# Two PSUM banks for the value sums, q and k turned in halves through one bank, the outcome's product on GpSimd, and no loop over heads

## What is computed

```python
q_bits = (einsum(q, proj) > 0)               # 6 bits for each token; k_bits alike
mask = q_bucket[..., :, None] == k_bucket[..., None, :]
scores = where(mask, q @ k.T / 8, -1e9)
attn = exp(scores - max); attn = attn / (sum(attn) + 1e-09)
x = attn @ v
h = maximum(maximum(x @ w1, x @ w2), x @ w3) @ w_out       # 512 -> 768 -> 512
return elu(h @ w_in) @ w_out2                              # 512 -> 2048 -> 512
```

## Time and profile before

| | before |
|---|---|
| median of 3 runs | 746.4 us (745.79 to 746.6) |
| the profiled execution | 744.61 us |
| its span, first to last instruction | 742.8 us |
| granted TensorE clock, mean | 0.989 |
| busy: PE, PEld, DVE, ACT, POOL | 97%, 83%, 51%, 57%, 50% |
| attention, until PE's first feed-forward matmul | 280.33 us |

### The profile page before, as it was taken

The page is one execution under the profiler, slowest core; times in us unless marked ns, Lnnn a source line. Parts: engine busy times, 40 slices in busy tenths (PEclk is TensorE's granted clock), DMA queues, the critical chain, the costliest instruction groups (busy, mean ns, idle before and its releaser), DMA issues.

```text
span 742.8 us, 10492 instructions
## 1 busy us (share of the span) xinstructions
PE 720.6 (97%) x3469; PEld 618.8 (83%) x3469; DVE 380.8 (51%) x615; ACT 424.5 (57%) x821; POOL 367.8 (50%) x333
## 2 busy tenths in 40 slices
PE   6899999999999979999999999999999999999998
PEld 5699999999998868888888888788888888888886
DVE  6768888988888844322222221243344433444333
ACT  4488989989898982221222121355555555555553
POOL 5377888888888871021110010254545444454442
PEclk8799999999999999999999999999999999999999
DMA  7656456464545000211000010133334333343331
GB/s 150 156 112 137 97 129 146 92 135 97 123 107 136 0 1 21 65 43 44 21 22 1 21 34 31 54 104 98 89 111 143 102 97 94 105 142 108 92 100 56
DMA packets 79317, 63.44 MB, mean 85 GB/s; under 512 B 29080, under 2 KB 68712, under 8 KB 79272
## 3 DMA queue, kind: packets, MB, share of 16 engines
q1 hardware_dynamic: 77416, 62.47, 33.0%
q10 hardware_dynamic: 1856, 0.40, 0.3%
HBM read 40.91 MB, written 3.15 MB: 59 GB/s over the span
## 4 chain that ended last, share of the span: by engine, by line
PE 60%; DVE 0%; ACT 0%; issue 0%
PE banks L781 14%; PE banks L783 14%; PE banks L782 14%; PE banks L1128 6%; PE banks L1124 6%; PE banks L1125 6%; DVE g_sb L1067 0%; DVE g_sb L1063 0%; DVE out_sb L1037 0%; ACT gh L1022 0%; ACT neg L1017 0%
## 5 line engine op out<-in xcount | busy, mean ns | idle before, releaser
L934 POOL TENSOR_TENSOR wl<-raw,wh 128x512 fp32r<-128x512 f32 (+2 forms) x104 | 143.5, 1398 | 301.7 <-ACT wh L950 301.7
L351 POOL TENSOR_TENSOR p_lo<-probs,p_hi 128x384 fp32r<-128x384 f32 x192 | 197.0, 1043 | 53.9 <-ACT p_hi L419 53.0
L781 PE MATMUL banks<-xh,wh 128*128 128x512 f32 x408 | 158.9, 389 | 0.5 <-PEq L126 0.5
L782 PE MATMUL banks<-xl,wh 128*128 128x512 f32 x408 | 158.8, 389 | 0.0
L783 PE MATMUL banks<-xh,wl 128*128 128x512 f32 x408 | 158.7, 389 | 0.0
L556 DVE TENSOR_REDUCE half_max<-banks 128x1 f32<-128x384 f32 x192 | 99.5, 547 | 27.7 <-PE banks L677 26.8
L418 ACT ACTIVATE probs<-banks 128x384 f32<-128x384 f32 x192 | 95.1, 495 | 26.2 <-PE banks L692 22.5
L419 ACT ACTIVATE p_hi<-banks 128x384 fp32r<-128x384 f32 x192 | 95.1, 496 | 0.0
L1063 DVE TENSOR_SCALAR g_sb<-banks 128x512 f32<-128x512 f32 x48 | 33.2, 692 | 120.1 <-ACT neg L1017 120.1
L781 PEld LDWEIGHTS banks<-xh,wh 128*128 128x128 f32 x408 | 76.6, 188 | 17.0 <-issue 0.9
L783 PEld LDWEIGHTS banks<-xh,wl 128*128 128x128 f32 x408 | 76.5, 188 | 16.0
(11 more groups left out here) (119 smaller groups left out, 1189.4 us busy)
## 6 DMA issues: line engine op xcount, KB each, us to landing
operands<-wh SPq DMA_DIRECT2D x36, 384.0 KB, 7.0
raw<-in_moe_w_in SPq DMA_DIRECT2D x48, 256.0 KB, 2.7
raw<-in_moe_w_out SPq DMA_DIRECT2D x48, 256.0 KB, 2.8
raw<-in_moe_w SPq DMA_DIRECT2D x18, 256.0 KB, 3.9
wl<-wh SPq DMA_DIRECT2D x9, 384.0 KB, 6.7
v_raw<-in_v SPq DMA_DIRECT2D x16, 192.0 KB, 2.5
out_dram<-out_sb SPq DMA_DIRECT2D x12, 256.0 KB, 2.1
q_raw<-in_q SPq DMA_DIRECT2D x15, 192.0 KB, 3.4
```

The source lines that it names most:

```text
L351: pool.tensor_tensor(p_lo[:, at, :], probs[:, step % RING, :], p_hi[:, at, :].bitcast(FP32), ALU.subtract).then_inc(pl_done, 1)
L781: pe.matmul(out, sh, mh, start=first, stop=False)
L782: pe.matmul(out, sh, ml, start=False, stop=False)
L934: pool.tensor_tensor(wl[:, j, at:at + cols], raw[:, j, at:at + cols], wh[:, j, at:at + cols].bitcast(FP32), ALU.subtract).then_inc(w_ready, 1)
```

## The change

1. `pv_ps` becomes two banks: the first half of every head goes into one, the second into the other. The first L706 of a half waits for the copies of the half before the last (the `o_read` counts go down by 2).
2. That bank comes from `misc`: from slot 1 on, q and k are turned, rounded, subtracted and projected through one bank (`single`), in halves of three transposes. PE turns q's halves at steps 0 and 3, k's at 5 and 8. ACT rounds each half (128x384) after the exponentials of the following step (1, 4, 6, 9). DVE subtracts the four halves before maxima 4, 7 and 11, and at the slot's end. Each transposing half waits until DVE has read the half before it; the projection of k waits for the bits of q.
3. The outcome's product moves from DVE (`divide`) to POOL, behind the last `p_lo` of the slot.
4. The loop is gone: all 22 slots are written out, and all counts are constants.

```diff
-TP_AT, HASH_AT = (0, 6), (3, 6)
+TP_AT, HASH_AT = ((0, 3), (5, 8)), (3, 6)
+LOW_AT = ((4, 7), (11, None))
...
-def all_slots(eng, emit):
-
-    for s in range(FIRST_SLOT, LOOP_FROM):
+def all_slots(emit):
+
+    for s in range(FIRST_SLOT, LAST_SLOT + 1):
         emit(Slot(s))
-    with eng.Fori(0, LOOP_TIMES) as g:
-        for j in range(GROUP):
-            emit(Slot(LOOP_FROM + j, g))
...
-        pv_ps = banks[:, RING + 2, :]
+        pv_ps = [banks[:, RING + 2 + i, :] for i in range(2)]
         misc = banks[:, RING + 3:, :]
+        single = banks[:, RING + 4, :]
...
+                if s.has_unit:
+                    pool.wait_ge(inv_done, s.count(2, -2))
+                    unit = (s.off - 2) % 4
+                    pool.tensor_tensor(x[:, unit, :], x[:, unit, :], inv[:, unit, :], ALU.mult).then_inc(x_done, 1)
...
+            def high_half(s, x, n, half):
+
+                if half == 0:
+                    act.wait_ge(t_half, s.count(1, n - 1))
+                else:
+                    act.wait_ge(t_ready, s.count(1, 3 + n))
...
+                act.activation(hi[x][:, half, :], single[:, 0:HALF], ACT.Copy
+                               ).then_inc(hi_done if half else hi_half, 1)
...
+                    for i, name in enumerate("qk"):
+                        if s.has_tp and s.off > FIRST_SLOT + 2 and step - 1 in TP_AT[i]:
+                            high_half(s, name, i + 1, TP_AT[i].index(step - 1))
...
+            def low_half(s, x, n, half):
+
+                if half == 0:
+                    dve.wait_ge(hi_half, s.count(1, n - 1))
+                else:
+                    dve.wait_ge(hi_done, s.count(1, 3 + n))
+                dve.tensor_tensor(lo[x][:, half, :], single[:, 0:HALF], hi[x][:, half, :].bitcast(FP32), ALU.subtract
+                                  ).then_inc(lo_done if half else lo_half, 1)
...
-                if s.has_unit:
-                    divide(s)
...
+            def transposes_half(s, x, n, half):
+
+                src = q_raw if x == "q" else k_raw
+                par = (s.off + 3) // 2 % 2
+                if half == 1:
+                    pe.wait_ge(lo_half, s.count(1, n - 1))
+                elif n == 1:
+                    pe.wait_ge(q_in[par], s.count(8, 56 - 16 * par))
+                    pe.wait_ge(bits_done, s.count(1, 3))
+                else:
+                    pe.wait_ge(k_in[par], s.count(8, 56 - 16 * par))
+                    pe.wait_ge(lo_done, s.count(1, 4))
+                for t in range(TH):
+                    last = pe.transpose(single[:, t * P:(t + 1) * P],
+                                        src[:, par, half * TH + t, :, :].rearrange("p a d -> p (a d)"), ident[:])
+                last.then_inc(t_ready if half else t_half, 1)
...
+                if s.off > FIRST_SLOT + 3 and n == 2:
+                    pe.wait_ge(bits_done, s.count(1, 3))
...
-                    wait(pe, o_read, s.count(4, -2 if step < LAG else 0))
+                    wait(pe, o_read, s.count(4, -4 if step < LAG else -2))
...
-                out, kept = pv_ps[:, 0:HALF], (STEPS * s.off + step - LAG) % KEPT
+                half = at // T
+                out, kept = pv_ps[half][:, 0:HALF], (STEPS * s.off + step - LAG) % KEPT
```

More of the change, by code:

```diff
@@ L99 @@
     has_hash = property(lambda s: not s.odd and -2 <= s.off <= HEADS - 4)
-def all_slots(eng, emit):
-    for s in range(FIRST_SLOT, LOOP_FROM):
+def all_slots(emit):
+    for s in range(FIRST_SLOT, LAST_SLOT + 1):
         emit(Slot(s))
-    with eng.Fori(0, LOOP_TIMES) as g:
-        for j in range(GROUP):
-            emit(Slot(LOOP_FROM + j, g))
[L109 to L115, removed]
 def wait(eng, sem, count):
-    if not isinstance(count, int) or count > 0:
+    if count > 0:
         eng.wait_ge(sem, count)
@@ L266, in emit @@
                 if s.has_max:
-                    head = held(sp, s.count(1, 1))
+                    head = s.count(1, 1)
                     wait(sp, vl_done, s.count(1))
@@ L277, in emit @@
                 if s.has_hash:
-                    split = s.count(1, 4) if s.g is None else sp.to_reg(s.count(1, 4))
+                    split = s.count(1, 4)
                     wait(sp, st_ready, s.count(STEPS) if s.off >= 2 else 0)
@@ L297, in emit @@
                         sp.wait_ge(consts, 14)
-                    both = s.count(1, 4) if s.g is None else sp.to_reg(s.count(1, 4))
+                    both = s.count(1, 4)
                     sp.wait_ge(bits_done, both)
@@ L371, in outcome @@
                 act.wait_ge(pv_ready, s.count(2, half - 1))
-                act.activation(x[rows, unit, :], pv_ps[0:D, 0:HALF], ACT.Copy).then_inc(o_read, 1)
-                act.activation(inv[rows, unit, :], pv_ps[D:P, 0:HALF], ACT.Copy).then_inc(o_read, 1)
+                act.activation(x[rows, unit, :], pv_ps[half][0:D, 0:HALF], ACT.Copy).then_inc(o_read, 1)
+                act.activation(inv[rows, unit, :], pv_ps[half][D:P, 0:HALF], ACT.Copy).then_inc(o_read, 1)
+            def high_half(s, x, n, half):
[3 more added lines that the diff above has]
+                    act.wait_ge(t_ready, s.count(1, 3 + n))
+                for a in range(2):
+                    act.wait_ge(spread1[a], s.count(SPREAD1 / 2, 1.5 * SPREAD1))
+                    act.wait_ge(spread2[a], s.count(SPREAD2 / 2, 1.5 * SPREAD2))
+                act.activation(hi[x][:, half, :], single[:, 0:HALF], ACT.Copy
+                               ).then_inc(hi_done if half else hi_half, 1)
             def high(s, x, n):
@@ L503, in take_bits @@
                 elif x == "q":
-                    last = dve.tensor_scalar(bits[:, 0, :], misc[:, 0, 0:HALF], 0.0, half_bits[:], ALU.is_gt,
+                    bank = misc[:, 0, :] if s.off == FIRST_SLOT + 3 else single
+                    last = dve.tensor_scalar(bits[:, 0, :], bank[:, 0:HALF], 0.0, half_bits[:], ALU.is_gt,
                                              ALU.subtract)
                 else:
-                    last = dve.tensor_scalar(bits[:, 1, :], misc[:, 1, 0:HALF], k_above[:], k_times[:], ALU.is_gt,
+                    last = dve.tensor_scalar(bits[:, 1, :], single[:, 0:HALF], k_above[:], k_times[:], ALU.is_gt,
                                              ALU.mult)
@@ L545, in emit @@
                         reciprocals(s, 1)
-                    if n == MAX_BEFORE[TP_AT[0] + 3] and s.has_tp and s.off != FIRST_SLOT + 2:
+                    if s.off == FIRST_SLOT and n == 0:
                         low(s, "q", 1)
+                    for i, name in enumerate("qk"):
+                        if s.has_tp and s.off > FIRST_SLOT + 2 and n in LOW_AT[i]:
+                            low_half(s, name, i + 1, LOW_AT[i].index(n))
                     if n == MAX_BEFORE[HASH_AT[0] + 1] and s.has_hash:
@@ L704, in weigh @@
                 pe.wait_ge(pl_done, s.count(STEPS, step - LAG + 1))
-                out, kept = pv_ps[:, 0:HALF], (STEPS * s.off + step - LAG) % KEPT
+                half = at // T
+                out, kept = pv_ps[half][:, 0:HALF], (STEPS * s.off + step - LAG) % KEPT
                 pe.matmul(out, v_hi[:, h % 2, kt, :], p_hi[:, kept, :], start=(kt == 0), stop=False)
                 pe.matmul(out, v_hi[:, h % 2, kt, :], p_lo[:, kept, :], start=False, stop=False)
-                pe.matmul(pv_ps[0:D, 0:HALF], v_lo[:, h % 2, kt, :], p_hi[:, kept, :], start=False, stop=False
+                pe.matmul(pv_ps[half][0:D, 0:HALF], v_lo[:, h % 2, kt, :], p_hi[:, kept, :], start=False, stop=False
                           ).then_inc(pv_step, 1)
@@ L713, in weigh @@
                         pe.wait_ge(empty_done, s.count(1, 1))
-                    half = at // T * HALF
-                    pe.matmul(out, total[:, h % 2, :], empty[:, h % 2, half:half + HALF], start=False, stop=True
+                    pe.matmul(out, total[:, h % 2, :], empty[:, h % 2, half * HALF:(half + 1) * HALF], start=False, stop=True
                               ).then_inc(pv_ready, 1)
@@ L727, in emit @@
                     for i, x in enumerate("qk"):
-                        if s.has_tp and step == TP_AT[i] and s.off != FIRST_SLOT + 2:
+                        if s.off == FIRST_SLOT and step == 6 * i:
                             transposes(s, x, i + 1)
+                        if s.has_tp and s.off > FIRST_SLOT + 2 and step in TP_AT[i]:
+                            transposes_half(s, x, i + 1, TP_AT[i].index(step))
                         if s.off == FIRST_SLOT + 2 and x == "q" and step == 3:
```

40 lines of the change are left out of this document (19 added, 21 removed).

## The result

The changed kernel takes 756.19 us (four runs, 755.26 to 757.9) beside 746.1 us of the kernel before on the same chip: a ratio of 1.0127, 95% interval 1.0106 to 1.0148. It is slower by 10 us. The forecast was 746.8 us and the range ended at 751.0.

What follows compares the result with a forecast made beforehand. PE, busy 97% of the span, was taken as the bound, with ACT, DVE and POOL near their limits mid-attention. +4.9 - 1.3 - 3.2 = +0.4 us on the profiled 744.61 gave 745.0, on the median 746.8; range 740.5 to 751 us.

Steps and rivals of the forecast that it cites:

- What is removed: Slots 1 to 12: two banks end PE's holds for the copies, 0.86 us a pair of slots, 5.2 us for six.
- Groups of transposes: On PE, four groups instead of two: about 0.09 us for each change of kind, 0.18 us a pair, 1.1 for six.
- The three waits of the halves: Odd slots, steps 3, 5 and 8: PE waits for the half before to be read, 0.2 to 0.3, 0.7, 0.4 us.
- w: Added waits of the halves in an odd slot, restarts included: 1.5 us, between 0.9 and 2.1; six make 9.0 us.
- the chain of step 5: k's first half: from PE's scores 4 to DVE's subtraction 2.5 us, PE's matmuls 1.8; a wait of 0.7, the surest.
- Neither is next in line there: Middle of attention: splitting adds 0.3 us a pair on ACT, with 2.2 of 30 us free, and as little on DVE.
- The longer chain: Rival, chance 0.20: `v_lo` and maxima ahead of the low half before maximum 4 double the first wait; 750.4 us.
- has lost its product: Argument for the covered-waits rival (chance 0.30; 741.4 us at w = 0.6): DVE's freed 0.94 us brings it sooner in each chain.
- cost nothing: POOL's added product, 1.04 us a slot, fits into 4.2 of 30 us free; if POOL were late, 0 to 1 us a pair.
- The loop: Writing out the loop over slots is worth 0 to 0.2 us; taken as 0.
- Slots 12 to 14: Without copy waits a slot falls from 15.0 to 14.3 or 14.5 us, limited by ACT and POOL; gain about 1.3 us.
- The end of attention: Slot 15 without PE's 2.11 us hold: POOL bounds, six `p_lo` 6.25 us plus 0.4 for DVE's subtraction; gain 3.2 us.

## Why the prediction was wrong

- **What is removed: right.** L706 no longer waits for the copies; the 0.86 us a pair are gone.
- **Groups of transposes: right.** 0.09 us for each change of kind, as taken.
- **The three waits of the halves: right in place, order and size.** Forecast 0.2 to 0.3, 0.7 and 0.4 us; lost start to start 0.29, 0.85 and 0.49, restart included, together 1.63. w was taken as 1.5. The argument that the chain of step 5 starts from PE itself was the sound one; the rounding one step sooner took nearly all three waits away, which shows that ACT's place in the step made them.
- **"Neither is next in line there": the step that failed.** It was said of ACT and DVE by their busy time, 28 and 26 of 30 us. But order decides, not share: DVE had 108.7 us of work in 133, less than before (109.5 in 124), and PE waited for its maxima 16 times between 40 and 290 us. `v_lo` is not mentioned in the part-by-part working at all; it was neither added nor moved by the change, and so its slack against `v_hi` and against the ring of maxima was not read. Both were in the trace of before: in its slot 8, `v_hi` ends at 153.63 and `v_lo` begins at 153.79, a slack of 0.16 us. The three terms 1.63, 0.18 and -0.86 make +0.95 us a pair; the maxima add 0.45, 0.96 and 0.10, 2.46 in all, against +2.35 measured. The prediction had put the maxima's term at nothing.
- **The longer chain, the rival priced 750.4 us, had the right place and too small a price.** It named DVE before maximum 4 with `v_lo` and the maxima ahead. It looked only at the halves of the odd slots. The wait falls on the ring of maxima itself, which is there in every slot, and it is the even slot that pays the larger part (0.96 of 1.41 us). `v_lo` one place later gives 9.8 us, 1.8 of them in slots 12 to 14; without this wait the time is 746.4 beside a forecast of 746.8. That close a match is in part luck: slots 12 to 14 then gain 2.0 us where 1.3 were forecast, and the end gains 2.3 where 3.2 were.
- **DVE "has lost its product": the freed 0.94 us did not help.** It stood for sooner turns of DVE. In the runs the product left DVE's queue at the slot's end but lengthened `v_lo` by 0.3 us (0.93 to 1.23) in its middle.
- **The product on POOL, "cost nothing": wrong in this order, right in another.** 2.9 us over the product on DVE, through DVE and not through ACT's wait for `probs`. With `v_lo` one place later it gains 2.7 us. The price of the operation itself, 1.04 us, was right (1.014). But the 0.94 us for L597 on DVE, with which the prediction compared it, is a mean over two kinds: in the middle of attention half of them take 0.54 to 0.56 us and the others 1.23 to 1.33, waiting beside POOL. Alone the product is 0.54 us on DVE, so POOL takes nearly twice as long, and the prediction's "nearly the same" was wrong.
- **The loop: right,** nothing.
- **Slots 12 to 14: 14.80 us instead of 14.3 to 14.5.** The same wait for maxima takes 0.8 and 0.5 us there; without it they take 13.9, so the limit by POOL that was argued, 14.2 us a slot, was too high: POOL is then busy for 27.29 of 27.81 us, 13.6 a slot.
- **The end of attention: 22.75 us after slot 14,** 2.3 us gained of 3.2. POOL sets the end, as argued, and its six `p_lo` begin as far behind slot 14 as forecast (14.45 us, forecast 14.37). But they take 7.44 us, not 6.65. DVE's large subtraction begins 0.01 us ahead of them, and the first `p_lo` takes 2.61 us: it waits for all of it, 1.6 us where 0.4 was put, of which the other five give back some at 0.97 us each. That is 0.8 of the missing 0.9 us. Of the gain itself a part is the clock: before, PE's hold of 2.11 us was followed by a fall, and the stretch had a mean granted clock of 0.93; after, it has 1.00.

```profile
285.35 1.74 DVE L613 TENSOR_TENSOR wl<-raw,wh 128x1536 fp32r<-128x1536 f32 x1
285.36 7.44 POOL L341 TENSOR_TENSOR p_lo<-probs,p_hi 128x384 fp32r<-128x384 f32 x6 [0.76 <-ACT p_hi L425]
```

- **The start.** PE waits 1.6 us once for a DMA of `bits` on the way to slot 1. The same distance varies from 15.2 to 20.3 us among the kernels here, with no edit near it; what sets it stays open. In the profiled executions shown it is 3.5 us longer after (18.65) than before (15.17); the odd slot's 1.87 us and the DMA wait of 1.6 make that up. The wait may be part of why these two are 13.3 us apart and the medians 10.1; the profiled run after is also the longest of its four.

## What to carry to other kernels

An edit that removes a wait lets the engine that had it run ahead, and what stops it next need not be the busiest engine; here it was the instruction that stands in front of the one it now waits for: read, for each ring, what is queued ahead of its release and how late that can start, also where the change touches none of it. A long operation on an in-order queue wants its place behind the releases of a short ring. And before a two-input operation is moved between DVE and POOL, look at when in POOL's operations those of DVE begin; moving one shifts all the others.

## What the runs showed of the hardware

DVE's `v_lo` reads two tensors in SBUF (the on-chip memory outside the banks), as POOL's subtractions and its product do, and they did not run side by side. From 100 to 240 us in all fourteen traces, each `v_lo` that began 0.03 to 0.88 us into a POOL operation ended 0.41 to 0.42 us after that operation's end (but for the one below), and POOL's next one, if it was ready, lasted 1.2 to 1.4 us instead of 1.01. DVE's reductions of a bank (0.55 us) and its subtractions with one input in a bank (0.55 us) kept their length beside POOL. The Trainium skill says this (SBUF — State Buffer, "SBUF: two separate sides"): the port pair is an exclusive lock held for a whole instruction, for DVE operations with two SBUF inputs too. The traces agree, also in the other direction: before, a product on DVE begun 0.02 us ahead of POOL's subtraction made that 1.39 us long.

```profile
151.50 0.54 DVE L597 TENSOR_TENSOR x<-x,inv 128x384 f32<-128x384 f32 x1
```

```profile
151.52 1.39 POOL L351 TENSOR_TENSOR p_lo<-probs,p_hi 128x384 fp32r<-128x384 f32 x1
```

Not expected was the `v_lo` of 5.22 us: begun 0.07 us after a POOL operation, it missed its turn at the ends of four operations and got in after the fifth, when POOL paused. It cost PE a stand of 2.52 us, and the lower clock behind it. Others that began as early (0.05 us, 1.37 us long) did not miss theirs, so the moment of the start alone does not explain it.
